# Second attention scores of the main tokens: two products of 64 rows a head become one of 128 rows over values padded with zeros

## The chip, the core and the metric

The kernel runs on one core of a Trainium2 chip. A core has TensorE (PE; its weight loads are listed apart as PEld), VectorE (DVE), ScalarE (ACT), GpSimd (POOL) and SyncE (SP), which issues the DMA transfers here, an on-chip memory (SBUF) of 128 partitions, and the accumulators of TensorE (PSUM), 128 partitions of 8 banks of 512 float32 values. The metric is the device time of one execution in microseconds.

## The reference

Three layers follow each other: a two-step attention over packed queries, a mixture of 8 experts that is computed densely with a balanced gate, and an MLP with a squared ReLU. Cut to what matters:

```python
def sm_attn(qq, kk, vv):                       # q, k, v: (4, 8, 576, 64); p: (4, 8, 32, 64)
    s = scale * np.matmul(qq, kk.transpose(0, 1, 3, 2))
    a = np.exp(s - np.max(s, axis=-1, keepdims=True))
    a = a / (np.sum(a, axis=-1, keepdims=True) + 1e-09)
    return np.matmul(a, vv)
p_packed = sm_attn(p, k, v)                    # 32 packed rows for each batch and head
out = sm_attn(q, p_packed, p_packed)           # every token attends to the 32 packed rows
# x: (2304, 512) from out; P: exp of x @ w_gate, normalised by rows and columns 8 times
for e in range(E):
    y += P[:, e:e+1] * (np.maximum(x @ w1[e], 0.0) @ w2[e])
r = np.maximum(y @ w_in, 0.0)
return (s * (r * r) + b) @ w_out
```

The change is in the second `sm_attn`, in its scores: the product of the queries of all 576 tokens with the 32 packed values, in each of 4 batches and 8 heads.

## The kernel before

The attention takes the first 75 us or so of the run; the experts and the MLP take the rest. It is written out by hand for the four batches. The order of TensorE's work there is a plain list of calls at the end of its block (`turn_q(0, 5)`, `scores2(0, 0)`, ...), and ScalarE and VectorE have lists of their own. A table `UNITS` names every set of transposes in order. They rotate over three PSUM banks, and before a set is turned TensorE waits until the one three places earlier has been copied away (`wait_evacuated`, `tr_free`).

Tokens: of the 576 tokens of a batch, 512 are main tokens and 64 the tail. A transposed query buffer `qT` holds two tokens for each column, one in partitions 0 to 63 and the other in partitions 64 to 127, each with its 64 head dimensions. So a chunk of 128 columns is 256 tokens: chunks 0 and 1 are the main tokens (r = 0 for the lower half of the partitions, r = 1 for the upper), chunk 2 is the tail of 32 columns. The packed values are needed in both halves. Therefore `turn_packed` turns a copy of them that holds every row twice, and ScalarE copies the result, 128 partitions of 256 columns (head, packed row), into `ppT` with one instruction (`packed_values`; all its copies are recorded under the line of the helper `copy`, L892).

`scores2(b, c)` computes the second scores of a chunk. For a main chunk it issues 16 products, r = 0 and r = 1 in turn. Each has 64 rows: the queries of one half as weights (64 x 128) and the 32 values of a head in the same half as the streamed operand. The two halves of the array work at the same time, and they write to two neighbouring banks: r = 0 goes up to the end of bank 4, r = 1 starts at the beginning of bank 5. Each streams its 32 columns four times (`copies = 4`, `to_broadcast`), so that 128 columns are written of which 32 stay in the end, as the order of the heads lets the right values overwrite the copies. For the last batch the banks are 4 and 6 (`LAST_S2B`). Float32 products of full precision are two records in the trace, each with a weight load. All products are recorded under the line of the helper `mm` (L1651), all transposes of the attention under L1671.

Around it: `scores2` waits for the packed values and the four sets of query transposes, and, from the second chunk on, for `s2_taken` of the chunk before, which VectorE raises when it has subtracted the maxima (`off_max2`, L1248 and L1249) and so freed the banks. Then come the exponential on ScalarE (`exp2`), the sums on VectorE (`inverse2`), the scaling on GpSimd (`normalise2`), and `turn_a` on TensorE. `packed_gates` multiplies `ppT` with the gate weights, `hi_of_packed` and `lo_of_packed` split its lower half for the experts' first products.

GpSimd starts with zeroing and filling the identity matrix and zeroing two buffers for the gates (L634, L635).

Of the kernel before, what the change touches and what calls it, by code (L numbers as in the profile page):

```python
# [12 lines left out]
P = 128  # L13
BANK = 512
# [4 lines left out]
def attention_moe_mlp(nc, q, k, v, p, w_gate, w1, w2, w_in, w_out, s_, b_, out):  # L19
# [6 lines left out]
    QUADS = H // 4  # L26
# [34 lines left out]
    with ExitStack() as ctx:  # L61
# [56 lines left out]
        p_twice = [sb(f"p_twice{i}", [P, QUADS, 2, D], scope=attn) for i in range(2)]  # L118
        pp = [sb(f"pp{i}", [P, QUADS, 2, D], scope=attn) for i in range(2)]
        pT = [sb(f"pT{i}", [P, QUADS * P], scope=attn) for i in range(2)]  # L120
        ppT = [sb(f"ppT{i}", [P, QUADS * P], scope=attn) for i in range(2)]
        stat = [sb(f"stat{i}", [P, 16], scope=attn) for i in range(2)]
        stat2 = [sb(f"stat2_{i}", [P, NC, 3, 2 * H], scope=attn) for i in range(2)]

# [78 lines left out]

        TR, S1B, S2B, PPB = (0, 1, 6), 2, 4, 7
        LAST_TR, LAST_S2B = (5, 4, 3), (4, 6, 4)

        GWB, LG, LGT = 7, (2, 3, 4, 5), 0
# [4 lines left out]
        COLB, COL_INVERSE, ROW_INVERSE = 7, 32, 64  # L214

        consts_ready, ones_ready = sem("consts_ready"), sem("ones_ready")
        v_in = sem("v_in")


# [215 lines left out]
            return found  # L435

        def s2_bank(b, c):
            return LAST_S2B[c] if b == B - 1 else S2B

        def scores2_of(b, c):
            at = s2_bank(b, c) * BANK + BANK - H * NPACK
            _, rows, groups = PARTS[c]
            return PS[0:rows, at:at + groups * NPACK].rearrange("s (h n) -> s h n", n=NPACK)

        def weights2_of(b, c):
# [180 lines left out]
        def _(pool):  # L629
            nc.gpsimd.memset(ident[:], 0.0).then_inc(consts_ready, 1)  # L630
            pool.wait_ge(consts_ready, 1)
            nc.gpsimd.affine_select(out=ident[:], in_=ident[:], compare_op=ALU.not_equal, fill=1.0, base=0,
                                    pattern=[[-1, P]], channel_multiplier=1).then_inc(consts_ready, 1)
            nc.gpsimd.memset(gw_both[:].bitcast(F32), 0.0).then_inc(wg_ready, 1)  # L634
            nc.gpsimd.memset(gw_high[:].bitcast(F32), 0.0).then_inc(wg_ready, 1)  # L635

# [253 lines left out]
        def _(act):  # L890
# [42 lines left out]

            def packed_values(b):

                evacuate("pp", b, 0, ppT[b % 2][:], lambda bank_: bank_[:, 0:QUADS * P])

            def hi_of_packed(b):

                wait_evacuated(act, [UNITS.index(("pp", b, 0))])  # L940
                copy(pp_parts[0:HALF, :, b * NPACK:(b + 1) * NPACK],
                     ppT[b % 2][0:HALF, :].rearrange("d (h n) -> d h n", n=NPACK)).then_inc(pp_hi_ready, 1)

            def p_part(b):
                evacuate("p", b, 0, pT[b % 2][:], lambda bank_: bank_[:, 0:QUADS * P])
# [44 lines left out]
            p_part(1)  # L990
            k_part(1, 2)
            k_part(1, 1)
            packed_values(0)
            k_part(1, 0)
            hi_of_packed(0)
# [209 lines left out]
        def _(dve):  # L1205
# [76 lines left out]
            def lo_of_packed(b):  # L1282
                dve.wait_ge(pp_hi_ready, b + 1)
                cols = slice(b * NPACK, (b + 1) * NPACK)
                nc.vector.tensor_tensor(
                    pp_parts[HALF:P, :, cols], ppT[b % 2][0:HALF, :].rearrange("d (h n) -> d h n", n=NPACK),
                    pp_parts[0:HALF, :, cols].bitcast(F32), ALU.subtract).then_inc(pp_split, 1)

            def gates_of_packed(b):
# [359 lines left out]
        def _(pe):  # L1649
# [98 lines left out]
            def scores2(b, c):  # L1748
                i, (col, tokens), n = b % 2, CHUNKS[c], b * NC + c
                wait_evacuated(pe, [UNITS.index(("pp", b, 0))] + [UNITS.index(("q", b, QUADS * c + Q))  # L1750
                                                                  for Q in range(QUADS)])
                if b == B - 1 and c == 1:
                    wait_evacuated(pe, range(LAST - 3, LAST))
                elif b == B - 1 and c == 2:
                    pe.wait_ge(s2_taken, n - 1)
                elif n:
                    pe.wait_ge(s2_taken, n)
                copies = 4 if c < NC - 1 else 1
                for step in range(H):
                    for r in range(2):  # L1760


                        h = step if r else H - 1 - step
                        rows = slice(r * HALF, (r + 1) * HALF)
                        weights_ = qT[i][rows, h, col:col + tokens]
                        values = ppT[i][rows, h * NPACK:(h + 1) * NPACK]
                        if c < NC - 1:
                            at = (s2_bank(b, c) + 1) * BANK + ((h * NPACK) if r else (h - H - copies + 1) * NPACK)
                            last = mm(PS[0:tokens, at:at + copies * NPACK].rearrange("s (o n) -> s o n", o=copies),
                                      weights_, values.unsqueeze(1).to_broadcast([HALF, copies, NPACK]))  # L1770
                        else:
                            at = (s2_bank(b, c) + 1) * BANK + (h - H) * NPACK
                            last = mm(PS[r * TAIL:(r + 1) * TAIL, at:at + NPACK], weights_, values)
                last.then_inc(s2_full, 1)

            def turn_a(b, c):
# [46 lines left out]
            def packed_gates(b):  # L1823
# [6 lines left out]
                for Q in range(QUADS):  # L1830
                    for hq in range(4):
                        h, rows = 4 * Q + hq, slice(hq % 2 * HALF, (hq % 2 + 1) * HALF)
                        last = mm(bank(GWB)[hq * NPACK:(hq + 1) * NPACK, Q * E:(Q + 1) * E],
                                  ppT[b % 2][rows, h * NPACK:(h + 1) * NPACK], wg_raw[rows, h // 2, :])
                last.then_inc(gw_full, 1)


# [434 lines left out]
```

## Time and profile before

| what | value |
| --- | --- |
| median of 3 runs | 1705.7 us (1705.32 to 1707.46) |
| the profiled execution's own time | 1704.49 us |
| its span, first to last instruction | 1702.7 us |
| TensorE busy | 1691.0 us, 99% |
| its weight loads busy | 1491.6 us, 88% |
| VectorE, GpSimd, ScalarE busy | 1253.8, 1253.5, 736.0 us |

In a line of the profile the names read "output<-inputs", with buffer numbers left out; `acc` and `second` are the memories in which the attention's work buffers of even and odd batches lie (`qT`, `e1`, `a2` and others). For a product, 64*128 64x128 means weights of 64 rows and 128 columns, and a streamed operand of 64 partitions with 128 columns. The durations of products include their way through the array and overlap; what one costs is seen in the distance of the starts. The time that stands in brackets is the engine's idle time before the instruction, with what ended it.

### The profile page before, as it was taken

How to read it: one execution, taken by the hardware profiler on the slowest of the kernel's cores; microseconds unless marked ns; L12 is line 12 of the kernel's file. 1: busy time of each engine (PE TensorE's matmuls, PEld its weight loads, DVE VectorE, ACT ScalarE, POOL GpSimd, SP SyncE). 2: the span in 40 equal slices, each digit the busy share in tenths (PEclk: the TensorE clock that was granted, in tenths of full speed). 3: DMA queues.
4: the chain of work that ended last, by engine and by line, in shares of the span. 5: the costliest groups of instructions: out<-in, count | busy, mean ns of one | idle time of the engine just before them, and what ended most of it. 6: DMA issues, size and time to landing. Idle time of an engine off the chain costs nothing.

```text
span 1702.7 us, 28100 instructions
## 1 busy us (share of the span) xinstructions
PE 1691.0 (99%) x10353; PEld 1491.6 (88%) x10353; DVE 1253.8 (74%) x2269; ACT 736.0 (43%) x1666; POOL 1253.5 (74%) x1384
## 2 busy tenths in 40 slices
PE   9999999999999999999999999999999999999999
PEld 7888888888888888888888888888888999889997
DVE  4846645787778787778787878787887677766776
ACT  5644466445444444445444545454532222232222
POOL 1256669987888888778888887888877985399650
PEclk9999999999999999999999999999999999999999
DMA  9431111111111211111112111111100011121101
GB/s 277 124 85 38 41 48 26 38 38 50 38 37 38 61 39 38 39 49 38 38 39 62 38 38 46 42 38 38 50 27 25 26 63 50 38 92 40 62 26 56
DMA packets 78390, 88.32 MB, mean 52 GB/s; under 512 B 8368, under 2 KB 63664, under 8 KB 78256
## 3 DMA queue, kind: packets, MB, share of 16 engines
q1 hardware_dynamic: 78256, 86.54, 18.9%
q8 instruction: 83, 1.36, 0.3%
q14 instruction: 51, 0.42, 0.1%
HBM read 81.81 MB, written 4.72 MB: 51 GB/s over the span
## 4 chain that ended last, share of the span: by engine, by line
PE 94%; POOL 2%; DMA 1%; ACT 1%; DVE 1%; SPq 1%; issue 0%; POOLq 0%; DVEq 0%
PE PS L1651 92%; PE PS L1671 2%; ACT g_raw L892 1%; DMA stage<-moe_w_dram 0%; POOL w_lo L643 0%; PE PS L1881 0%; DMA k_tail<-k_dram 0%; SPq L514 0%; DVE acc L1352 0%; POOL span_late L732 0%; POOL w_hi L641 0%; POOL recombined L716 0%; SPq L538 0%; POOL sums_of_a L724 0%; SPq L531 0%
## 5 line engine op out<-in xcount | busy, mean ns | idle before, releaser
L1651 PE MATMUL PS<-w_hi,h_hi 128*128 128x512 f32 x1440 | 565.7, 393 | 1.2 <-DVE h_lo L1583 0.6
L1651 PE MATMUL PS<-w_lo,h_hi 128*128 128x512 f32 x1440 | 563.4, 391 | 0.0
L1651 PE MATMUL PS<-w_hi,h_lo 128*128 128x512 f32 x1440 | 560.6, 389 | 0.0
L1357 DVE SCALAR_TENSOR_TENSOR acc<-PS,gate,acc 128x512 f32<-128x512 f32 x504 | 378.3, 751 | 178.9 <-PE PS L1651 178.9
L892 ACT ACTIVATE g_raw<-PS 32x256 f32<-32x256 f32 x992 | 373.3, 376 | 12.8 <-PE PS L1651 0.8
L1651 PEld LDWEIGHTS PS<-w_hi,h_lo 128*128 128x128 f32 x1440 | 270.4, 188 | 58.6
L1651 PEld LDWEIGHTS PS<-w_hi,h_hi 128*128 128x128 f32 x1440 | 270.8, 188 | 51.1 <-DVE h_lo L1583 1.1
L1651 PEld LDWEIGHTS PS<-w_lo,h_hi 128*128 128x128 f32 x1440 | 270.9, 188 | 45.8
L1108 ACT ACTIVATE h_hi<-PS 128x576 fp32r<-128x576 f32 x216 | 129.0, 649 | 303.4 <-DVE PS L1493 303.4
L1651 PE MATMUL PS<-a_parts,g_slots 128*128 128x288 f32 x1296 | 225.1, 295 | 0.2 <-POOL g_slots L764 0.2
L1651 PEld LDWEIGHTS PS<-a_parts,g_slots 128*128 128x128 f32 x1296 | 195.7, 188 | 9.6 <-POOL g_slots L764 0.6
L643 POOL TENSOR_TENSOR w_lo<-stage,w_hi 128x1024 fp32r<-128x1024 f32 (+1 forms) x94 | 190.6, 2028 | 7.5
L1493 DVE TENSOR_TENSOR PS<-PS,snaps 128x288 f32<-128x288 f32 x432 | 177.3, 456 | 0.1
L1493 DVE TENSOR_TENSOR snaps<-PS,snaps 128x288 f32<-128x288 f32 x324 | 148.4, 458 | 38.8 <-ACT snaps L892 16.8
L892 ACT ACTIVATE snaps<-PS 128x288 f32<-128x288 f32 (+2 forms) x134 | 55.1, 411 | 268.7 <-PE PS L1651 268.6
L1352 DVE TENSOR_TENSOR acc<-PS,acc 128x512 f32<-128x512 f32 x180 | 123.9, 688 | 56.5 <-PE PS L1651 55.5
L1651 PE MATMUL PS<-sums_of_a,g_slots 128*128 128x288 f32 x972 | 164.2, 295 | 0.6 <-ACT snaps L892 0.6
L1516 DVE SCALAR_TENSOR_TENSOR h_lo<-PS,h_hi 128x576 fp32r<-128x576 f32 x216 | 161.5, 748 | 0.0
L764 POOL TENSOR_TENSOR g_slots<-g_sums,g_slots 128x512 fp32r<-128x512 f32 x108 | 139.8, 1294 | 8.5
L1651 PEld LDWEIGHTS PS<-sums_of_a,g_slots 128*128 128x128 f32 x972 | 140.7, 188 | 0.8 <-ACT snaps L892 0.8
L752 POOL CAST g_slots<-g_raw 128x384 fp32r<-128x384 f32 x108 | 54.8, 507 | 112.2 <-ACT g_raw L892 92.4
L658 POOL TENSOR_TENSOR w_lo<-stage,w_hi 128x1024 fp32r<-128x1024 f32 x48 | 115.5, 2406 | 3.8
(181 smaller groups left out, 2315.4 us busy)
## 6 DMA issues: line engine op xcount, KB each, us to landing
stage<-moe_w_dram SPq DMA_DIRECT2D x96, 512.0 KB, 4.8
stage<-moe_w_in_dram SPq DMA_DIRECT2D x32, 256.0 KB, 2.8
stage<-moe_w_out_dram SPq DMA_DIRECT2D x16, 512.0 KB, 3.6
k_raw<-k_dram SPq DMA_DIRECT2D x8, 512.0 KB, 6.3
q_raw<-q_dram SPq DMA_DIRECT2D x8, 512.0 KB, 5.8
v_raw<-v_dram SPq DMA_DIRECT2D x8, 512.0 KB, 6.7
out_dram<-acc SPq DMA_DIRECT2D x16, 256.0 KB, 3.7
p_twice<-p_dram SPq DMA_DIRECT2D x8, 64.0 KB, 4.7
```

The costliest lines, as they stand in the source:

```text
L643: nc.gpsimd.tensor_tensor(lo, src, hi.bitcast(F32), ALU.subtract).then_inc(w1_ready, 1)
L658: nc.gpsimd.tensor_tensor(w2_lo[par][:], stage2[:], w2_hi[par][:].bitcast(F32), ALU.subtract).then_inc(w2_ready, 1)
L752: nc.gpsimd.tensor_copy(hi[:, G11:GS1, :], raw[:, 1:4, :]).then_inc(g_step, 1)
L764: nc.gpsimd.tensor_tensor(lo[:, GS1:BLOCKS, :], g_sums[:], hi[:, GS1:BLOCKS, :].bitcast(F32), ALU.subtract).then_inc(g_split, 1)
L892: return nc.scalar.activation(dst, src, ACT.Copy)
L1108: nc.scalar.activation(h_hi[:, f, b % 2 * S:(b % 2 + 1) * S].rearrange("p (i n) -> p i n", i=2), bank(HB + 2 * f, 2 * BANK).rearrange("p ( ...
L1352: return nc.vector.tensor_tensor(dst, y, dst, ALU.add)
L1357: return nc.vector.scalar_tensor_tensor(out=dst, in0=y, scalar=share, in1=dst, op0=ALU.mult, op1=ALU.add)
L1493: nc.vector.tensor_tensor(dst, bank(at, SPAN), term, ALU.add).then_inc(joined, 1)
L1516: nc.vector.scalar_tensor_tensor(out=h_lo[:, f, cols].rearrange("p (i n) -> p i n", i=2), in0=bank(HB + 2 * f, 2 * BANK).rearrange("p (i n ...
L1651: return nc.tensor.matmul(dst, lhsT, rhs, start=start, stop=stop)
L1671: last = nc.tensor.transpose(bank(unit_bank(unit))[0:m_, c0:c0 + k_], src, ident[0:k_, 0:k_])
```

## The change

The packed values get a layout with zeros: `ppT` is now 128 partitions x 8 heads x 2 x 32, in which r = 0 has values only in partitions 0 to 63 and r = 1 only in 64 to 127. The other two quarters are zeroed once, at the start, by GpSimd, and ScalarE writes the two filled quarters with two copies of 64 partitions. With that, a head of a main chunk is one product: weights of 128 rows (both tokens of a column) and 64 streamed columns, of which the first 32 come out as the scores of r = 0 and the last 32 as those of r = 1. They go to one bank, 256 columns for each r. Chunks alternate between banks 4 and 5, and the wait for `s2_taken` refers to the chunk before last. The copies of the streamed columns are gone. The tail keeps its products of 64 rows and 32 columns.

```diff
-        ppT = [sb(f"ppT{i}", [P, QUADS * P], scope=attn) for i in range(2)]
+        ppT = [sb(f"ppT{i}", [P, H, 2, NPACK], scope=attn) for i in range(2)]
...
-        TR, S1B, S2B, PPB = (0, 1, 6), 2, 4, 7
+        TR, S1B, S2B, PPB = (0, 1, 6), 2, (4, 5), 7
...
+        zeros_ready = sem("zeros_ready")
...
         def s2_bank(b, c):
-            return LAST_S2B[c] if b == B - 1 else S2B
-
+            return LAST_S2B[c] if b == B - 1 else S2B[(b * NC + c) % 2]
...
         def scores2_of(b, c):
-            at = s2_bank(b, c) * BANK + BANK - H * NPACK
             _, rows, groups = PARTS[c]
+            at = s2_bank(b, c) * BANK + (BANK - H * NPACK if c == NC - 1 else 0)
...
+            for i in range(2):
+                nc.gpsimd.memset(ppT[i][:], 0.0).then_inc(zeros_ready, 1)
...
             def packed_values(b):
-                evacuate("pp", b, 0, ppT[b % 2][:], lambda bank_: bank_[:, 0:QUADS * P])
+                unit = UNITS.index(("pp", b, 0))
+                for r in range(2):
+                    rows = slice(r * HALF, (r + 1) * HALF)
+                    done = copy(ppT[b % 2][rows, :, r, :],
+                                full(unit)[rows, 0:QUADS * P].rearrange("d (h n) -> d h n", n=NPACK))
+                done.then_inc(evacuated(unit), 1)
...
-                     ppT[b % 2][0:HALF, :].rearrange("d (h n) -> d h n", n=NPACK)).then_inc(pp_hi_ready, 1)
+                     ppT[b % 2][0:HALF, :, 0, :]).then_inc(pp_hi_ready, 1)
...
+            act.wait_ge(zeros_ready, 2)
             packed_values(0)
...
-                elif n:
+                elif b == B - 1:
                     pe.wait_ge(s2_taken, n)
-                copies = 4 if c < NC - 1 else 1
-                for step in range(H):
+                elif n >= 2:
+                    pe.wait_ge(s2_taken, n - 1)
+                for h in range(H):
+                    if c < NC - 1:
+                        last = mm(bank(s2_bank(b, c))[0:tokens, :].rearrange("s (r h n) -> s r h n", r=2, h=H)[:, :, h, :],
+                                  qT[i][:, h, col:col + tokens], ppT[i][:, h, :, :])
+                        continue
                     for r in range(2):
...
-                        h = step if r else H - 1 - step
                         rows = slice(r * HALF, (r + 1) * HALF)
-                        weights_ = qT[i][rows, h, col:col + tokens]
-                        values = ppT[i][rows, h * NPACK:(h + 1) * NPACK]
-                        if c < NC - 1:
-                            at = (s2_bank(b, c) + 1) * BANK + ((h * NPACK) if r else (h - H - copies + 1) * NPACK)
-                            last = mm(PS[0:tokens, at:at + copies * NPACK].rearrange("s (o n) -> s o n", o=copies),
-                                      weights_, values.unsqueeze(1).to_broadcast([HALF, copies, NPACK]))
-                        else:
-                            at = (s2_bank(b, c) + 1) * BANK + (h - H) * NPACK
-                            last = mm(PS[r * TAIL:(r + 1) * TAIL, at:at + NPACK], weights_, values)
+                        at = (s2_bank(b, c) + 1) * BANK + (h - H) * NPACK
+                        last = mm(PS[r * TAIL:(r + 1) * TAIL, at:at + NPACK], qT[i][rows, h, col:col + tokens],
+                                  ppT[i][rows, h, r, :])
                 last.then_inc(s2_full, 1)
```

`lo_of_packed` and `packed_gates` read `ppT` at its new places in the same way. The order of instructions on all engines stays as it was, apart from these places. On TensorE, from the query transposes ahead of chunk (0,0) to those ahead of chunk (0,1); names with their buffer numbers, the shape is that of the output. Before:

```order
L1671 MATMUL PS<-ident,q_raw0 128x128 x4
L1651 MATMUL PS<-ppT0,acc 128x128 x16
L1671 MATMUL PS<-ident,q_raw0 128x128 x4
L1651 MATMUL PS<-second,pT1 32x288 x8
L1671 MATMUL PS<-ident,q_raw0 128x128 x4
L1671 MATMUL PS<-ident,k_raw0 128x128 x4
L1671 MATMUL PS<-ident,q_tail0 128x32 x4
L1651 MATMUL PS<-ppT0,acc 128x128 x16
```

After, with all line numbers 10 higher:

```order
L1681 MATMUL PS<-ident,q_raw0 128x128 x4
L1661 MATMUL PS<-ppT0,acc 128x2x32 x8
L1681 MATMUL PS<-ident,q_raw0 128x128 x4
L1661 MATMUL PS<-second,pT1 32x288 x8
L1681 MATMUL PS<-ident,q_raw0 128x128 x4
L1681 MATMUL PS<-ident,k_raw0 128x128 x4
L1681 MATMUL PS<-ident,q_tail0 128x32 x4
L1661 MATMUL PS<-ppT0,acc 128x2x32 x8
```

The row of 16 products has become one of 8, whose output is 128 partitions x 2 x 32; what stands around it has not moved. On ScalarE, from the copy of the second batch's packed queries (`pT`) to the split of the packed values (`pp_parts`). Before:

```order
L892 ACTIVATE pT<-PS 128x256
L892 ACTIVATE second<-PS 128x4x32 x2
L892 ACTIVATE second<-PS 128x4x128
L892 ACTIVATE ppT<-PS 128x256
L892 ACTIVATE second<-PS 128x4x128
L892 ACTIVATE pp_parts<-ppT 64x8x32
L892 ACTIVATE second<-PS 128x4x128 x2
```

After:

```order
L896 ACTIVATE pT<-PS 128x256
L896 ACTIVATE second<-PS 128x4x32 x2
L896 ACTIVATE second<-PS 128x4x128
L896 ACTIVATE ppT<-PS 64x8x32 x2
L896 ACTIVATE second<-PS 128x4x128
L896 ACTIVATE pp_parts<-ppT 64x8x32
L896 ACTIVATE second<-PS 128x4x128 x2
L926 ACTIVATE second,stat<-PS,stat 128x576
```

The copy into `ppT` is two copies of 64 partitions, 8 heads and 32 columns. On TensorE at the end of attention, from the third batch's last transposes to the tail of batch 3. Before:

```order
L1671 MATMUL PS<-ident,pp1 128x128 x2
L1651 MATMUL PS<-stage1,pp_parts 32x256 x16
L1671 MATMUL PS<-ident,acc 128x128 x4
L1671 MATMUL PS<-ident,acc 128x64 x2
L1651 MATMUL PS<-ppT1,second 128x128 x32
L1651 MATMUL PS<-ppT1,second 32x32 x16
```

After:

```order
L1681 MATMUL PS<-ident,pp1 128x128 x2
L1661 MATMUL PS<-stage1,pp_parts 32x256 x16
L1681 MATMUL PS<-ident,acc 128x128 x4
L1681 MATMUL PS<-ident,acc 128x64 x2
L1661 MATMUL PS<-ppT1,second 128x2x32 x16
L1661 MATMUL PS<-ppT1,second 32x32 x16
```

The two chunks follow each other with 16 products instead of 32, between transposes of 64 rows and the tail's products.

## Rows read from the trace of the kernel before

**Rows 1.** the page: busy times, and the clock in 40 slices
```profile
PE 1691.0 (99%) x10353; PEld 1491.6 (88%) x10353; DVE 1253.8 (74%) x2269; ACT 736.0 (43%) x1666; POOL 1253.5 (74%) x1384
...
PEclk9999999999999999999999999999999999999999
```

**Rows 2.** chain of waits in order of time; start us, us, what
```profile
18.31 1.69 PE PS L1671 x14
...
81.00 0.60 SPq L552
...
293.35 1000.91 PE PS L1651 x5511
```

**Rows 3.** lines by shape, 0 to 90 us
```profile
L1651 PE MATMUL PS<-ppT,acc 64*128 64x128 f32 x128 | 8.2, 278 | 0.0
```

**Rows 4.** timeline of PE, chunk (0,0); start us, us, engine, line
```profile
23.13 0.27 PE L1671 MATMUL PS<-ident,q_raw 128*128 128x128 f32 x1
23.33 0.37 PE L1651 MATMUL PS<-ppT,acc 64*128 64x128 f32 x1
...
25.11 0.28 PE L1651 MATMUL PS<-ppT,acc 64*128 64x128 f32 x2
25.32 0.33 PE L1671 MATMUL PS<-ident,q_raw 128*128 128x128 f32 x1
```

**Rows 5.** timeline of the weight loads (PEld) at 140 us
```profile
139.95 0.30 PEld L1651 LDWEIGHTS PS<-col_sum,ones 128*128 128x128 f32 x2 [0.26 <-DVE col_sum L1322]
140.16 0.19 PEld L1651 LDWEIGHTS PS<-w_hi,h_hi 128*128 128x128 f32 x1
140.28 0.19 PEld L1651 LDWEIGHTS PS<-w_lo,h_hi 128*128 128x128 f32 x1
```

**Rows 6.** timeline of PE, products of 128 rows and 288 columns
```profile
75.22 1.85 PE L1651 MATMUL PS<-a_parts,g_parts 128*128 128x288 f32 x12
```

**Rows 7.** timeline of PE, transposes of 128 rows, then products
```profile
1495.28 0.49 PE L1881 MATMUL PS<-ident,acc 128*128 128x128 f32 x3
1495.53 0.48 PE L1651 MATMUL PS<-w_hi,h_hi 128*128 128x512 f32 x1
1495.84 0.39 PE L1651 MATMUL PS<-w_lo,h_hi 128*128 128x512 f32 x1
```

**Rows 8.** timeline of PE at chunk (0,1), 32-row transposes on both sides
```profile
27.57 0.44 PE L1671 MATMUL PS<-ident,q_tail 32*128 32x32 f32 x4
27.94 0.37 PE L1651 MATMUL PS<-ppT,acc 64*128 64x128 f32 x1
...
29.49 0.50 PE L1651 MATMUL PS<-ppT,acc 64*128 64x128 f32 x6
...
29.92 0.43 PE L1671 MATMUL PS<-ident,k_tail 32*128 32x32 f32 x4
```

**Rows 9.** timeline of PE, 16-row transposes, then products of 128 rows
```profile
108.31 0.40 PE L1855 MATMUL PS<-ident,acc 16*128 16x16 f32 x4
108.64 0.39 PE L1651 MATMUL PS<-w_hi,pp_parts 128*128 128x256 f32 x1
108.86 0.28 PE L1651 MATMUL PS<-w_lo,pp_parts 128*128 128x256 f32 x1
```

**Rows 10.** timeline of PE, the last chunks with their tails
```profile
70.88 4.41 PE L1651 MATMUL PS<-ppT,second 64*128 64x128 f32 x95
```

**Rows 11.** timeline of ACT behind the first packed values
```profile
19.86 0.38 ACT L892 ACTIVATE ppT<-PS 128x256 f32<-128x256 f32 x1
20.13 0.60 ACT L892 ACTIVATE second<-PS 128x512 f32<-128x512 f32 x1
...
21.60 0.60 ACT L892 ACTIVATE second<-PS 128x512 f32<-128x512 f32 x1 [0.58 <-PE PS L1671]
```

**Rows 12.** lines by shape, 0 to 90 us, GpSimd's zeroing
```profile
L634 POOL MEMSET gw_both<- 128x1024 f32 x1 | 1.0, 952 | 0.0
```

**Rows 13.** timeline of PE, the opening products
```profile
1.06 4.52 PE L1651 MATMUL PS<-ones 128*128 128x128 f32 x20 [1.06 <-DVE ones L1214]
```

More of the change, by code:

```diff
@@ L1285, in lo_of_packed @@
                 nc.vector.tensor_tensor(
-                    pp_parts[HALF:P, :, cols], ppT[b % 2][0:HALF, :].rearrange("d (h n) -> d h n", n=NPACK),
+                    pp_parts[HALF:P, :, cols], ppT[b % 2][0:HALF, :, 0, :],
                     pp_parts[0:HALF, :, cols].bitcast(F32), ALU.subtract).then_inc(pp_split, 1)
@@ L1833, in packed_gates @@
                         last = mm(bank(GWB)[hq * NPACK:(hq + 1) * NPACK, Q * E:(Q + 1) * E],
-                                  ppT[b % 2][rows, h * NPACK:(h + 1) * NPACK], wg_raw[rows, h // 2, :])
+                                  ppT[b % 2][rows, h, hq % 2, :], wg_raw[rows, h // 2, :])
                 last.then_inc(gw_full, 1)
```

## The prediction

> **What bounds the kernel now.** I read the busy table and the slices first: TensorE is busy for 99% of the span, VectorE for 74%, and the granted clock is at its upper level (2.4 GHz) in all 40 slices [rows 1]. The reader should see that no other engine can be the bound on average, but also that "99%" says nothing of how densely products follow each other. So I went on to the chain of waits in order of time. From 18.31 us, when the last early transfer landed, it runs on TensorE alone until 81.00 us, with no other engine between; there the SyncE queue takes over, released by TensorE, for the next expert's weights; and from 293.35 us it is TensorE for 1000.91 us [rows 2]. All eight main products of the second scores lie between 23.3 and 74.6 us, so in the part where TensorE is the chain. What they get faster moves everything behind them, the weight transfer issued at 81.00 us too.
>
> Third, the lines by shape up to 90 us. A product of full precision is two records, each with a weight load. The 8 main chunks x 8 heads x 2 halves x 2 records = 256 products of form 64*128 64x128 (half under acc, half under second), 0.278 us each [rows 3], and as many loads. These durations overlap, so I do not add them up; I work with starts. Last I looked at single instructions. A product behind a change of tile shows its wait as a longer duration: 0.37 instead of 0.27 us. I call start plus that excess the effective start.
>
> **The present cost of one chunk**, at its first place (batch 0, chunk 0, with transposes of 128 rows on both sides) [rows 4]: the last transpose starts at 23.13, the first pair effectively at 23.33 + 0.10 = 23.43, the last pair at 25.11, the next transpose effectively at 25.32 + 0.06 = 25.38. That is 0.30 in, 15 intervals of 0.112 = 1.68, and 0.27 out: 2.25 us.
>
> **The new cost of the same chunk.** It has 8 products of 128 rows and 64 columns, that is 16 records, one behind the other; before, 16 pairs. What the columns need is halved (256 column steps a record become 128, 0.053 us at 2.4 GHz), so now the weight load sets the interval. Where a product of this kind (full precision, 128*128 weights) has only 8 columns, loads start at 139.95, +0.11 (two take 0.30, one 0.19), 140.16 and 140.28: 0.11 to 0.12 apart [rows 5]. I take S = 0.111 us. So 15 intervals are 1.67 us: the stream itself gains 0.015, nothing much, though half of the products are gone. That the load is hidden behind the product before it is shown by 12 products of 288 columns in 1.85 us [rows 6]: less the last one's duration of about 0.30, 0.14 each, while load (0.107) and columns (0.120) in a row would need 0.23.
>
> The gain is at the edges. In: a transpose of 128*128 starts last at 1495.28 + 0.49 - 0.27 = 1495.50, the product of 128*128 weights behind it effectively at 1495.53 + (0.48 - 0.39) = 1495.62 [rows 7]: 0.12 instead of 0.30. Out: a transpose's load is about half as long, and transposes with 128 weight columns and little to stream are some 0.06 apart (four in 0.43, of which the last one's duration is 0.22; the first a little late) [rows 8]: 0.06 instead of 0.27. Together 0.12 + 1.67 + 0.06 = 1.85, a gain of 0.40 us.
>
> By place, where only the neighbours differ. (0,0) and (1,1), 128 rows on both sides: 0.39 at the edges each, 0.78. (1,0) and (2,1), narrower tiles ahead, 128 rows behind: the exit gives 0.21. The entry gives nothing: from 32 rows it takes 27.94 + 0.10 - (27.57 + 0.44 - 0.22) = 0.25 now [rows 8], and from 16 rows to 128*128 weights 108.64 + (0.39 - 0.28) - (108.31 + 0.40 - 0.21) = 0.25 as well [rows 9]. So 0.42 for the two. (0,1) and (2,0), 32 rows on both sides: the tile still changes on both; the way out is now 29.92 - (29.49 + 0.50 - 0.27) = 0.20 [rows 8], of which 0.11 is the last product's columns, and 0.05 of them remain: 0.06 each, 0.12. (3,0) and (3,1) follow each other, with 64-row transposes ahead and 64-row tails behind, 95 records of scores in 4.41 us [rows 10]: they have no full change of rows now and get two. In 0.25 instead of 0.11, out 0.14 instead of 0.20, some 0.03 of stream: -0.05. The other six streams: 6 x 0.015 = 0.09. Sum: 0.78 + 0.42 + 0.12 - 0.05 + 0.09 = 1.36, say 1.3 us.
>
> **The rest of the change.** ScalarE copies the packed values in two pieces instead of one. The next copy starts 0.27 us behind such a copy (19.86 to 20.13) [rows 11], and I take as much for a copy of half the partitions with as many columns, so each batch costs ScalarE another 0.27 us. Behind the first one it has 0.58 us of idle time ahead of 21.60 [rows 11], so the delay ends there; the keys that it copies in between (from 20.40 instead of 20.13) are done at 21.00, where TensorE turns other sets meanwhile. The cost is nothing while that cover holds, and at most 4 x 0.27 = 1.1 us without it. The two zeroings on GpSimd stand ahead of two of 0.95 us for twice the columns [rows 12], so add about 1 us near 3 us of the run, wanted at 19.86: nothing. The gates and the tails read the values at another stride with the same rows and columns: nothing. VectorE reads as many scores as before, in one bank instead of two halves; TensorE's wait for it now refers to the chunk before last. No product of the scores waits for VectorE in the profile, so this frees nothing; it only guards against a wait coming in as the chunks draw together.
>
> The profiled execution took 1704.49 us for its span of 1702.7; minus 1.3 it would be 1703.2. It is 1.2 below the median of the three runs, 1705.7, to which the forecast refers: **1704.4 us**. The interval S is the one unknown that matters, with 6 x 15 + 31 = 121 of them. Low end 0.06, the interval of transposes whose load is one pass [rows 8]: 121 x 0.05 = 6 us more gain, 1698.3. High end 0.14, the interval of [rows 6], for the case that it is set by the load and its latency and not by the 288 columns: 121 x 0.029 = 3.5 us lost, net +2.2, 1707.9. I stay at 0.111 because it is the row with this precision, these rows and these columns.
>
> The Trainium skill has a rule against this change ("TensorE: Matmul & The Clock Gate", Part 3, The mechanism): a weight load runs beside products in flight only when its row group differs. The new products all use all rows, so by it load and columns would add up. The trace disagrees by the 0.14 us of [rows 6], products of 128 rows throughout; no run yet shows it for full precision at 64 columns.
>
> The same page (Part 2, Back-to-back issue gap) gives about 81 ns for each pair of load and product at 128 columns. As an estimate by that page S would be at most 0.081 and the gain 3.6 us larger. The loads of [rows 5] stand against it.
>
> **Rivals.** (A) Loads and columns add up: S = 0.107 + 0.053 = 0.16. Then 121 x 0.049 = 5.9 us are lost against 1.3 gained: 1710.3, slower. For it: only that no row has this exact form; against it [rows 6]. The sign turns at S = 0.122. Chance 0.04.
> (B) The clock falls. The columns' share of each interval drops from 0.107 of 0.112 to 0.053 of 0.111, in 1.8 us stretches, and 3.4 us at the end of attention. At the lower level (1.2 GHz) the opening's 20 products took 4.52 us, 0.21 apart [rows 13], twice the 0.11 of transposes with as many columns [rows 7]. One fall as long as that costs 2.1 us (1706.5), three cost 6.3 (1710.7). Against it: between 5.6 and 16 us there are mostly transposes with gaps, and the clock stays up [rows 1]. One fall is enough to turn the sign. Chance 0.08.
> (C) The edges gain, but ScalarE's four longer copies are waited for, or S lies between 0.12 and 0.14: 1705.5 to 1707.9. The margin behind the first copy is 0.58 us [rows 11], so a partial stall is the worst that the rows allow. Chance 0.18.
> (D) S well below 0.1, the loads hidden better than in [rows 5]: 1698 to 1702. Chance 0.05.
> Forecast 0.65.
>
> **Numbers.** This measurement tells nothing below 0.2%, 3.4 us. Faster by more than that needs D, or a lucky sum: 0.08. Slower by more needs A or several falls of B: 0.08. The rest, 0.84, lies within. The range holds the forecast, C, one fall of B and the scatter of the runs before (1705.32 to 1707.46): 1701.8 to 1707.6.
>
> **What would show it.** 128 products of form 128*128 128x64 with loads of 0.19 and an interval of 0.11; 1.85 instead of 2.25 us from the transpose ahead of (0,0) to the one behind; (0,1) and (2,0) hardly changed; the SyncE piece at 79.7 instead of 81.00; eight copies into ppT. Wrong: an interval of 0.13 or 0.16; a slice with the clock below 9; an idle TensorE behind the first copies; or a span that keeps its length although the edges shrank, which would mean that something other than TensorE held 18 to 81 us.

## The result, and the profile after

The changed kernel takes 1711.0 us (median of 13 runs, 1706.7 to 1714.2) against 1705.3 (13 runs, 1704.0 to 1707.5): ratio 1.0030, 95% interval 1.0023 to 1.0037. It is slower, and the forecast of 1704.4 us with its range up to 1707.6 is wrong. Of all timed runs below one, of e2_copies2, stands apart with 2070.3 us at a mean granted clock of 0.752: its median counts it, its ratio does not.

The products themselves did what the prediction said. The timeline of TensorE (start, duration, engine, line, operation, tile, count) at chunk (0,0) of the changed kernel answers to [rows 4]:

```profile
23.52 0.66 PE L1681 MATMUL PS<-ident,q_raw 128*128 128x128 f32 x4
24.01 1.90 PE L1661 MATMUL PS<-ppT,acc 128*128 128x64 f32 x16
25.75 0.60 PE L1681 MATMUL PS<-ident,q_raw 128*128 128x128 f32 x4
```

Sixteen records in 1.90 us, of which the last one's duration is about 0.22: 15 intervals of 0.112 us. Single starts in the trace say 23.90 for the last transpose ahead, so 0.11 in, and 25.75 for the next one: 1.84 us where it was 2.19 (start to start, 23.13 to 25.32 in [rows 4]). Where [rows 3] had 128 such records with 256 column steps, there are half as many (busy us, mean ns, idle ahead), loads included:

```profile
L1661 PE MATMUL PS<-ppT,acc 128*128 128x64 f32 x64 | 7.9, 277 | 0.0
L1661 PEld LDWEIGHTS PS<-ppT,acc 128*128 128x128 f32 x64 | 7.5, 192 | 0.1
```

The page, though, has a slice with the clock below 9 ([rows 1] has none), and TensorE is busy for 5.5 us more with 128 records fewer:

```profile
PE 1696.5 (99%) x10225; PEld 1496.8 (88%) x10225; DVE 1253.8 (73%) x2269; ACT 735.5 (43%) x1670; POOL 1251.9 (73%) x1386
...
PEclk9899999999999999999999999999999999999999
```

The second slice is 42.7 to 85.5 us of the run. By tens of us (window, its length, busy time of PE, PEld, DVE, ACT and POOL with their counts, granted clock, transfers, GB/s) the changed kernel shows two things, an idle TensorE and then half the clock:

```profile
20.00:30.00 10.00, 9.87 (x122) 7.90 (x120) 5.56 (x15) 7.36 (x17) 0.24 (x1) 1.00 1.02 316
30.00:40.00 10.00, 8.41 (x155) 6.65 (x154) 5.96 (x15) 3.65 (x9) 1.85 (x2) 0.89 0.82 230
40.00:50.00 10.00, 10.00 (x59) 8.29 (x59) 3.31 (x6) 4.73 (x13) 0.00 (x0) 0.50 0.51 159
50.00:60.00 10.00, 9.87 (x197) 7.76 (x196) 7.22 (x23) 6.60 (x16) 1.99 (x3) 0.93 0.39 106
```

The timeline of TensorE names the place. It is not at the changed products but in those of batch 1's values, between the first and the other seven records of one group that no semaphore parts:

```profile
34.83 0.65 PE L1661 MATMUL PS<-v_raw,second 128*32 128x64 f32 x32
35.41 0.24 PE L1661 MATMUL PS<-v_tail,second 64*32 64x64 f32 x1
37.24 0.31 PE L1661 MATMUL PS<-v_tail,second 64*32 64x64 f32 x7 [1.59 <-issue]
37.48 0.51 PE L1681 MATMUL PS<-ident,p_twice 128*128 128x128 f32 x2
...
44.31 3.67 PE L1661 MATMUL PS<-ppT,second 128*128 128x64 f32 x16
```

From load to load 1.83 us pass, where two loads of such a group are 5 to 10 ns apart otherwise. "issue" means that nothing in the profile was waited for. The clock stood at its lower level (1.2 GHz) from 37.72 to 51.37 us, 13.65 us. Chunk (1,0) lies in it: 3.67 us for what takes 1.90 elsewhere. The chain's long piece of [rows 2], which began at 293.35, begins 6.90 us later and is as long as before, so everything was lost ahead of it:

```profile
300.25 1000.91 PE PS L1661 x5511
```

The sum for the profiled execution: idle 1.7, half of 13.65 is 6.8, a start that is 0.7 later (first keys of batch 1 turned at 18.99, not 18.31), less about 1.0 at the eight chunks and 0.5 for a short pause of the kernel before near 66.5 us that is gone: 7.7, where the spans say 6.9.

One more row of the changed kernel's page bears on what follows, the transfers by queue (packets, MB, share):

```profile
q8 instruction: 82, 1.34, 0.3%
```

The trace has each of the 82 with 16,384 bytes. It has 20,992 records of TensorE's sequencer and array, 82 times 256; in the kernel before 21,248, 83 times 256, and 83 such transfers (in all 14 profiles of this study the count of transfers is that of whole 256s). So these are TensorE's own instructions, 256 of 64 bytes at a time. One of them started at 34.82 us, 0.6 us ahead of the pause.

### The profile page after: what moved, and what is told of

The parts are those of the page before. It is cut to its first block, busy times and chain, and to the rows that moved or that the text cites. A ratio compares the mean times of both kernels' runs of the same rounds, so it can differ in the third digit from the quotient of the medians.

```text
span 1709.6 us, 27851 instructions
## 1 busy us (share of the span) xinstructions
PE 1696.5 (99%) x10225; PEld 1496.8 (88%) x10225; DVE 1253.8 (73%) x2269; ACT 735.5 (43%) x1670; POOL 1251.9 (73%) x1386
## 4 chain that ended last, share of the span: by engine, by line
PE 95%; POOL 2%; DVE 1%; ACT 1%; issue 0%; DMA 0%; SPq 0%; POOLq 0%; DVEq 0%
PE PS L1661 93%; PE PS L1681 2%; ACT g_raw L896 1%; PE PS L1887 0%; DMA k_raw<-k_dram 0%; POOL w_lo L647 0%; DVE acc L1362 0%; POOL span_late L736 0%; POOL recombined L720 0%; POOL sums_of_a L728 0%; DVE a_parts L1572 0%; POOL w_lo L662 0%; DVE PS L1588 0%; POOL w_hi L645 0%; DVE h_lo L1593 0%
```

## The experiments

Two theories. C: the clock falls because each interval of the new products has half the columns (rival B of the prediction). F: TensorE waited for its instructions, since the change takes 16 records and 16 loads, 32 instructions, out of each chunk and so moves the points at which a new block of 256 is needed; the clock fell behind the wait. To take the start's scatter out of the profiles I give a stretch beside the times: from the first keys of batch 1 to the last gate products, in the kernel before 58.69 us:

```profile
18.31 0.43 PE L1671 MATMUL PS<-ident,k_tail 32*128 32x32 f32 x4
...
77.00 0.31 PE L1651 MATMUL PS<-wg_raw,ppT 64*32 64x8 f32 x16
```

In the changed kernel it is 64.96. The kernel before was timed anew beside each set of runs, and every ratio refers to its own set: 1706.2 us (35 runs) for e1 to e4, 1706.5 (24) for e5 to e8, 1705.8 (35) for e9 to e12.

**e1_twice: the changed kernel with the columns of before.**

```diff
-   ... [:, :, h, :], qT[i][:, h, col:col + tokens], ppT[i][:, h, :, :])
+   ... [:, :, h:h + twice, :], qT[i][:, h, col:col + tokens],
+   ppT[i][:, h, :, :].unsqueeze(2).to_broadcast([P, 2, twice, NPACK]))   # twice = 2, heads 0 to 6
```

> Changed kernel, but heads 0 to 6 of a main chunk stream every value column twice (128 columns instead of 64; the second copy is overwritten by the next head). Loads, records and their interval stay (0.11 us). Theory C (the clock fell because the halved columns leave the array less active): the clock stays at its upper level in all slices, the changed edges remain, and the time is 1704.0 us (1.3 below the 1705.3 of before). Theory F (the clock fell because TensorE waited 1.83 us for its instructions at 35.41 us): nothing changes, the clock still falls for some 10 to 14 us and the time stays near 1711.

Measured 1710.2 us (11 runs), ratio 1.0025 [1.0016, 1.0034], stretch 62.16. The same pause at the same instruction:

```profile
37.22 0.24 PE L1661 MATMUL PS<-v_tail,second 64*32 64x64 f32 x1
39.05 0.31 PE L1661 MATMUL PS<-v_tail,second 64*32 64x64 f32 x7 [1.59 <-issue]
```

and a fall from 41.69 to 48.52. Columns do not prevent it. Chunk (0,0) takes 1.84 us from transpose to transpose as in the changed kernel, so the interval is 0.112 us with 128 columns as with 64.

**e2_copies2: the kernel before with half its columns.**

```diff
-                copies = 4 if c < NC - 1 else 1
+                copies = 2 if c < NC - 1 else 1
```

> Kernel before, but the columns of a main chunk are streamed twice instead of four times: products of 64 rows and 64 columns, the same number of instructions as before. Theory C: the load sets the interval of a pair (0.11 us), the clock falls for 10 to 14 us in the attention, 1711 to 1713. Theory F: the instructions are those of before, no longer wait, the clock stays up, 1705.

Measured 1704.8 us (12 runs; the ratio of 11 is 0.9991 [0.9982, 1.0000]), the clock at its upper level in every slice, although TensorE paused twice (0.71 us from load to load near 20.4, 0.89 near 66.8). C has fallen on both sides.

**e3_shift: the changed kernel with 128 more instructions in the opening.**

```diff
+            for n in range(32):
+                mm(PS[0:32, PPB * BANK:PPB * BANK + 8], ones[:, 0:32], ones[:, 0:8])
```

> Changed kernel with 32 more products of 32 weight columns and 8 streamed columns in the opening, ahead of the first data: 128 more instructions, so that the places where TensorE's instructions are fetched move. Theory F: no wait of 1.8 us at the same products, and the clock stays up (1704) or falls elsewhere. Theory C: the clock falls as in the changed kernel, 1711, whether such a wait is there or not.

Measured 1706.4 us (11 runs), ratio 1.0006 [0.9997, 1.0015]; the small products made the opening 1.5 us longer. The pause in the values' products is gone. The profiled execution has another one, and this has a plain reason:

```profile
38.68 0.65 PE L1683 MATMUL PS<-ident,acc 128*128 128x128 f32 x4
41.13 0.81 PE L1683 MATMUL PS<-ident,q_raw 128*128 128x128 f32 x4 [1.80 <-DMA q_raw<-q_dram]
```

The clock fell behind it too (41.51 to 48.33), although TensorE had waited here for data and not for instructions.

**e4_layout: the zeroed layout, its memsets and ScalarE's two copies, with the products, banks and waits of before.**

```diff
-                    if c < NC - 1:
-                        last = mm(bank(s2_bank(b, c))[0:tokens, :]. ...
+                        values = ppT[i][rows, h, r, :]
+                        if c < NC - 1:
+                            last = mm( ... weights_, values.unsqueeze(1).to_broadcast([HALF, copies, NPACK]))
```

> Layout with zeros, zeroing and the two copies on ScalarE of the changed kernel, but products, banks and waits of the kernel before (64 rows, four times 32 columns). Both theories: clock up, 1705.3. If ScalarE's longer copies stall TensorE: up to 1.1 us more, 1706.4.

Measured 1706.2 us (10 runs), ratio 1.0003 [0.9994, 1.0012], stretch 59.06 with the chunks at 2.19 and 2.14 us as before. The interval runs from 1.0 us faster to 2.0 us slower; the profile shows no cost: 0.3 us of the 0.4 by which the stretch is longer is the pause at record 2241, 0.89 us from load to load instead of 0.61.

Before the next runs I laid the blocks of 256 over the traces. Every pause of TensorE with "<-issue" in the timelines up to 110 us, in these and the later profiles, comes at record 449, 961, 1217, 1729, 1985 or 2241 (counted by start, give or take two): 193 plus a multiple of 256. Worked out from the records (us; "entered": TensorE begins the block ahead; "landed": start plus duration of the transfer; pause from load to load):

```
kernel    record  entered  transfer starts  landed  pause from, us   work again  since landing
changed      961    30.88            34.82   35.70  35.41  1.83           37.24           1.54
e1_twice     961    32.69            36.76   37.64  37.22  1.83           39.05           1.40
before      2241    62.62            64.44   65.65  66.49  0.61           67.10           1.45
before       961    28.38            28.35   29.27  none          (entry at 34.52)        5.24
e9 (below)   961    32.28            36.31   37.19  none          (entry at 39.69)        2.50
```

In the row of the kernel before with no pause 256 instructions took 6.1 us, and their successors' transfer started at once. In the last row the transfer started as late as in the changed kernel, 4.0 us after the entry, but the 256 ahead took 7.4 us. In the changed kernel two chunks lie ahead of this boundary, so it stands 64 instructions further down the program, in the products of batch 1's values; these issue 80 records and 80 loads in 1.7 us. The 256 ahead of it took 4.5 us, and the transfer started 3.9 us after the entry. The keys and values of the next batches were being transferred then; that they are what delays it is likely, but no run varied them alone. F in numbers, for the first 80 us of all profiles: the transfer of a block starts from 0.4 us before to 6.1 us after the entry of the block ahead (once 7.7), lasts 0.9 to 1.5 us ahead of a pause, and the block can be used 1.3 to 1.6 us after landing. Where TensorE gets through 256 instructions faster, it stands. The entry, read from the records' starts, is not itself what releases the transfer: after 100 us, where 256 instructions take over 20 us and few data are moved, the transfers start up to 4.2 us before it.

**e5_after_shift: the changed kernel, boundaries 64 instructions further up.**

```diff
-            for n in range(10):
+            for n in range(8):
                 mm(bank(PPB, P), ones[:], ones[:])
+            for n in range(18):
+                mm(PS[0:32, PPB * BANK:PPB * BANK + 8], ones[:, 0:32], ones[:, 0:8])
```

> The changed kernel with 64 more TensorE instructions in the opening: 8 instead of 10 products of 128*128 by 128, and 18 products of 32 weight columns by 8 columns (each product is two loads and two records), which by the earlier shift run (64 such records 1.5 us) last as long as before. Theory F (TensorE gets its instructions in blocks of 256; a block is transferred only when the one before it has been entered, 0.4 to 6 us later, and can be used 1.4 to 1.6 us after it has landed): the boundary that fell into the products of the tail values at 35.4 us moves 64 instructions up the stream, and no block between 30 and 110 us is gone through in less than 6.5 us (4.4 before). So no pause inside a product group, no fall of the clock behind it, and the 1.3 us of the forecast come out: 1703.5 to 1705, 0.999 of the kernel before. Theory C (the clock falls because the product columns are halved): the columns are as in the changed kernel, so it falls again, 1709 to 1711. A third view, that the pause comes from the zeroed layout or the banks at this place of the program: pause and fall as in the changed kernel.

Measured 1706.1 us (11 runs), ratio 0.9996 [0.9987, 1.0005], 5 us less than the changed kernel; no pause, no fall, stretch 57.19:

```profile
21.61 0.43 PE L1683 MATMUL PS<-ident,k_tail 32*128 32x32 f32 x4
...
78.80 0.31 PE L1661 MATMUL PS<-wg_raw,ppT 64*32 64x8 f32 x16
```

The time is 1 us above what I expected, and the profile puts that on the opening that I edited: with two full products fewer there the clock rose only at 13.98 us (5.32 before), and the stretch began 3.3 us late.

**e6_before_shift: the kernel before, boundaries 184 instructions further up** (5 full and 51 small products in the opening; no edit elsewhere).

> The kernel BEFORE with 184 more TensorE instructions in the opening (5 instead of 10 full products and 51 small ones, about 0.2 us longer than before), the second scores untouched. Theory F: a block boundary now falls into the same products of the tail values of batch 1 (near 35 to 36 us) in which the changed kernel stood still, and the block ahead of it is gone through in about 4 us. A transfer that starts 3 to 4 us after the entry, lasts 0.9 and can be used 1.5 later needs 5.5 to 6.5: a pause of 1 to 2.5 us inside the group with no semaphore, and a clock at its lower level for 6.8 or 13.7 us soon after it, 1708 to 1713 in most runs. Theory C: nothing of the second scores is changed, so no fall: 1705 to 1706.5.

Measured 1714.2 us (5 runs), ratio 1.0048 [1.0034, 1.0061]: no faster than the changed kernel, with the second scores untouched.

```profile
41.22 0.30 PE L1651 MATMUL PS<-v_tail,second 64*32 64x64 f32 x5
43.59 0.30 PE L1651 MATMUL PS<-v_tail,second 64*32 64x64 f32 x3 [2.08 <-issue]
```

The pause (2.34 us from load to load) stands in the same group as in the changed kernel, as F said; the clock fell from 45.67 to 49.08. The stretch is 62.80: 58.69 + 2.3 + 1.7. The rest of the 7.7 us lies again in the opening, where the clock rose at 18.36 and the stretch began at 24.43.

**e7_pause: the kernel before with a written pause.**

```diff
+        pause = sem("pause")
...
+                        if b == 1 and Q == 1 and j == RUN:
+                            for step in range(7):
+                                mm(PS[0:32, 6 * BANK - 8:6 * BANK], ones[:, 0:32], ones[:, 0:8]).then_inc(pause, 1)
+                                pe.wait_ge(pause, step + 1)
```

> The kernel BEFORE with a pause written into the products of batch 1's values (near 35 us): seven products of 32 by 8 columns into an unused corner of a bank, each of which TensorE waits for before it goes on; about 0.25 to 0.3 us each, 1.8 to 2.1 us together. It tells how much of the loss is the pause and how much the clock. If a pause of this length is enough to lower the clock: 1.9 us plus a fall of 6.8 us (3.4 lost) or 13.7 us (6.8 lost): 1711 to 1714. If the pause must be an instruction wait or belongs to the changed products: only the 1.9 us, 1707.5 to 1708, clock at the upper level throughout.

Measured 1710.7 us (8 runs), ratio 1.0030 [1.0020, 1.0041]. The time is that of "pause and a fall", and it misleads. The profile has no fall behind the pause:

```profile
37.99 1.95 PE L1652 MATMUL PS<-ones 128*32 128x8 f32 x14
40.00 0.32 PE L1652 MATMUL PS<-v_tail,second 64*32 64x64 f32 x8
```

```profile
71.13 0.65 PE L1652 MATMUL PS<-v_raw,second 128*32 128x64 f32 x30
72.71 0.27 PE L1652 MATMUL PS<-v_raw,second 128*32 128x64 f32 x2 [0.93 <-issue]
```

Stretch 62.01: 58.69, 1.95 for the pause, and more waiting for instructions behind it (1.2 us at record 2241, 0.5 at 1729), since its 28 instructions moved the boundaries. The clock had fallen in the opening instead (8.71 to 15.54), behind 1.88 us of waiting for keys. Here 1.95 us of small products, one about every 0.28 us, were not followed by a fall, in the one profile that there is. How much of the loss is the pause and how much the clock, which this run was to measure, it did not tell.

**e8_before_shift2: the kernel before, 112 instructions, meant as a control** (7 full and 31 small products).

> The kernel BEFORE with 112 more TensorE instructions in the opening (7 full products and 31 small ones). It is the control for the shift of 184: again only the boundaries move, but to where the shortest block between 30 and 110 us takes 5.2 us instead of 4.5 as before and 3.8 with 184. Theory F: no pause above 0.5 us in a group, no fall, and the 0.6 us of idle time that the kernel before has near 66.5 us goes too: 1704.5 to 1706. If added instructions or another opening were themselves what costs the time: as with 184, 1708 or more.

Measured 1708.8 us (11 runs, 1706.2 to 1713.5), ratio 1.0014 [1.0005, 1.0023]; neither of the two. There was a pause, at the next boundary:

```profile
40.37 0.70 PE L1651 MATMUL PS<-acc,pT 64*32 64x288 f32 x13
42.35 1.17 PE L1651 MATMUL PS<-acc,pT 64*32 64x288 f32 x3 [1.28 <-issue]
```

My condition was too coarse: the block took 5.2 us, but its transfer started 4.5 us after the entry, so TensorE stood for 1.9 us from load to load (1.28 between its products, which have 288 columns here). The clock fell from 42.08 to 48.90. The mechanism holds, the bound "5.2 us is enough" does not: with a start as late as this it would have needed 6.9.

**e9_after_fill64 and e12_after_fill80: the changed kernel, shifted without touching the opening; e11_before_fill64: the same 16 products in the kernel before; e10_changed_again: no edit.**

```diff
+            def small(count):
+                for _ in range(count):
+                    mm(PS[0:32, PPB * BANK:PPB * BANK + 8], ones[:, 0:32], ones[:, 0:8])
...
 scores1:
+                if n == 1:
+                    small(10)        # e12: 12
...
 turn_e:
+                if b == 0 and n == 1:
+                    small(6)         # e12: 8
```

> The changed kernel with 64 more TensorE instructions again, but the opening is left alone (10 full products; the shift before it lowered their number, and the clock rose only at 14.0 us and the first keys of batch 1 were turned at 21.6 instead of 18.3 us). The 16 small products stand where TensorE waits for ScalarE in both kernels: 10 ahead of the second first-score products (0.7 to 1.0 us idle), 6 ahead of the turning of the second part of the weights (0.54 us idle). Theory F: no pause inside a group between 30 and 60 us, no fall of the clock, from the first keys of batch 1 to the gates at 77 us 57.2 us as in the shift before (58.7 in the kernel before, 65.0 in the changed one), and since the start is no longer late, 1703.5 to 1705, ratio 0.9985 to 0.9995. If the pause is bound to the changed products or their banks: 1709 to 1711.

> The changed kernel itself, on the same chip as the other three. Theory F: pause of about 1.8 us in the tail products near 35 us at the same instruction, a fall of 6.8 or 13.7 us behind it; 1708 to 1713. A chance event of one chip or one day would show here as a trace without either, and 1703 to 1705.

> The kernel BEFORE with the same 16 small products at the same two places. Theory F: the same fillers that heal the changed kernel hurt this one, because its boundaries stand elsewhere: the block entered near 51 us holds 256 instructions that take 4.0 us (4.5 without the fillers), while a transfer needs 2.7 to 5 us to start, 1.0 to 1.3 to land and 1.45 until it can be used: a pause of 1 to 2.5 us near 55 us, and in many runs a fall of the clock behind it: 1706.5 to 1711. If the fillers themselves were what makes a kernel faster (a warmer clock, say): 1703.5 to 1705.5.

> The changed kernel with 80 more instructions (12 and 8 small products at the same two places). By Theory F a version next to a good one is good as well: the shortest block takes 6.5 us with 48, 64 and 80 alike: no pause over 0.6 us in a group between 30 and 70 us, 1703.5 to 1705.5. If the gain of 64 was luck, this one scatters over 1704 to 1711.

Measured against 1705.8 (35 runs) of the kernel before: e9 1704.3 us, ratio 0.9994 [0.9986, 1.0003]; e10 1711.4, 1.0028 [1.0019, 1.0037]; e11 1709.0, 1.0020 [1.0012, 1.0029]; e12 1706.3, 1.0004 [0.9995, 1.0013]. The same fillers take 7 us from the changed kernel and add 3 to the one before. e10 repeats the pause of the changed kernel to the instruction (2.10 us; clock down 40.97 to 51.21, stretch 64.25):

```profile
37.25 0.24 PE L1661 MATMUL PS<-v_tail,second 64*32 64x64 f32 x1
39.35 0.31 PE L1661 MATMUL PS<-v_tail,second 64*32 64x64 f32 x7 [1.86 <-issue]
```

e11 stands where F said it would, near 55 us (2.24 us from 52.45; clock down 55.92 to 59.34, stretch 62.02):

```profile
52.17 0.66 PE L1675 MATMUL PS<-ident,k_raw 128*128 128x128 f32 x4
54.79 0.41 PE L1675 MATMUL PS<-ident,pp 128*128 128x128 f32 x2 [1.97 <-issue]
```

e12 has none, and in its profile the values' products are whole and the stretch is 57.30 (e9: 57.28):

```profile
34.60 0.65 PE L1661 MATMUL PS<-v_raw,second 128*32 128x64 f32 x32
35.19 0.32 PE L1661 MATMUL PS<-v_tail,second 64*32 64x64 f32 x8
35.43 0.44 PE L1685 MATMUL PS<-ident,p_twice 128*128 128x128 f32 x2
```

e12 scatters over 1703.1 to 1709.6 all the same, which I had called the sign of luck. Each timed run has a mean granted clock, and it sorts them. Of the 24 runs of the changed kernel (13 and 11) none has 1.000. Of the 35 runs of the kernel before that were timed beside e9 to e12 21 have it, median 1704.9; of the 22 of e9 and e12, 12 have it, 1703.1 to 1704.4, median 1704.0. The others lie higher by what their clock says. At least one such fall lies in the opening: e9's profiled execution (1708.4, clock 0.997) has 2.0 us of waiting for keys at 7.98 us and the lower clock from 9.18 to 19.42, and no pause behind it. Whether that is so in e12's slower runs no trace shows.

## Why the prediction was wrong

**The products: right.** 16 records a chunk, loads of 0.192 us, S = 0.112 against 0.111 (of the four loads of [rows 5] the last two belong to products of 512 columns, so the row was near the case and not the case itself; the value held). Rivals A and D have fallen: loads of 128 rows in full precision do run beside the products ahead of them: e1 doubles the columns and the interval stays. That is against the rule of the Trainium skill that the prediction weighed ("TensorE: Matmul & The Clock Gate", Part 3, The mechanism), "only when row_grp differs"; the same section also lets a load go ahead when it targets a "background weight buffer", which would fit, but no run here shows that buffer. The 81 ns of its Part 2 do not appear; the trace says 0.112 us.

**The edges: right in kind, a third too large.** Start to start, in e12 against the kernel before: (0,0) and (1,1) 2.188 to 1.842, 0.35 each where I had 0.40; (1,0) and (2,1) 2.137 to 1.986 and 2.089 to 1.937, 0.15 each for 0.21; (0,1) and (2,0) 2.138 to 2.082, 0.06 as forecast; the last two chunks with their tails 4.40 to 4.49 (70.81 to 75.22 and 69.78 to 74.27), 0.09 lost where I had 0.05. That is 1.0 us, not 1.36. The term that was mis-sized is the edge: I added a longer duration's excess to the start of the transpose behind the chunk, and the trace shows no such delay there. The stretch says about the same: 58.7 less the pause of 0.5 near 66.5 us, to 57.3, leaves 0.9.

**ScalarE, GpSimd, banks, waits: right as far as e4 resolves it.** No cost shows in its profile; rival C has fallen. No SyncE piece at 79.7 could be seen: in e12 the chain stays on TensorE there.

**The failed step** is the first one: "What they get faster moves everything behind them". It takes the part from 18 to 81 us as a row of durations on one engine that can only shift. The number of instructions was a term of its own: 64 fewer in two chunks moved the boundary at record 961 from a place where the 256 ahead of it took 6.1 us to one where they took 4.5, into the middle of the values' products. That cost 1.8 to 2.1 us of standing and, behind it, 6.8 to 13.7 us at half the clock (e1, e10, the changed kernel), against a gain of 1.0. With 64 fillers ahead, which put this boundary back where it was, both are gone.

**Rival B had the symptom and the wrong cause.** It priced three falls at 1710.7, close to the 1711.0 measured, but it tied the fall to the columns, which e1 and e2 refute, and had 0.08. I gave "the clock falls" as little because TensorE was 99% busy in the page; I did not ask what could make it idle with no semaphore in play. The page had the answer in a line that I passed over, the queue with 83 instruction transfers, and a pause of 0.46 us "<-issue" at 67.21 us in the kernel before:

```profile
66.31 0.43 PE L1671 MATMUL PS<-ident,q_tail 32*128 32x32 f32 x4
67.21 0.31 PE L1671 MATMUL PS<-ident,second 64*128 64x64 f32 x2 [0.46 <-issue]
```

The Trainium skill ("Advanced Engine Details and Errata", ISA Cache) says that instructions are cached in lines of 16 KB, 256 instructions, and that there are two of them. The trace agrees with the line (16,384 bytes, pauses at 256 instructions' distance) and with two in use. For TensorE the section also gives a larger cache, 128 KB; these traces give no sign of more than one block ahead of the one in work.

**The best version.** The changed kernel with 64 filler instructions, 1704.3 us, beats the changed one by 7 us. Against the kernel before its interval reaches from 0.14% faster to 0.03% slower; a gain does not show in the medians of all runs. Among the runs at full clock it does, 0.8 to 0.9 us (1704.0 against 1704.9), but these are picked by their clock, and about 0.5 of it is the short pause near 66.5 us that the fillers moved away, not the products. The 1.0 us that the products gain is read from the profiles; no time on record shows it by itself.

## What to carry to other kernels

Count the instructions of the engine that bounds the kernel as well as its time: where 256 of them pass faster than the next 256 arrive (5.2 us were too few in e8, 6.1 enough in the kernel before), a change that removes instructions anywhere ahead can place the boundary there. Look for idle time with "issue" as its releaser inside a group that has no wait, and compare its instruction numbers modulo 256 before blaming the edited lines. If the new version loses time far from the edit, shift it by a few dozen cheap instructions where the engine idles anyway, and shift the old one too: if the sign follows the shift, the edit is not at fault.

## What the runs showed of the hardware that was not expected

- TensorE waits for its own instructions: 15 pauses of 0.4 to 2.3 us in 11 of 14 profiles, every one at 193 plus a multiple of 256 records, with work again 1.3 to 1.6 us after a 16 KB transfer had landed.
- The clock fell to 1.2 GHz at every stretch of 1.8 to 2.3 us from one weight load to the next (seven in the main part, four in the opening of e1, e7, e9 and e10), between 0.8 us before work began again and 3.0 us after; behind stretches of up to 1.3 us, measured in the same way, it did not. How long it stayed down differed for the same pause: 6.8 us in e1, 10.2 in e10, 13.7 in the changed kernel; behind longer pauses elsewhere it was 3.4 (e6, e11). I have no explanation for which one comes.
- In the opening with its 10 full products the clock rose between 4.0 and 7.0 us, with 8 full and 18 small ones at 14.0, with 5 and 51 at 18.4. With 7 and 31 it rose at 4.5 and fell again at 7.95 without an idle stretch over 0.6 us. Each of the last three is one profile, and no rule comes out of them.
